# Moving the second layer's down weights out of the second stage of a two-layer split-precision kernel

## The chip, the cores and the metric

The kernel runs on one core of one Trainium2 chip. The time is device microseconds of one execution; three executions of the kernel before are shown, and one more was taken with the hardware profiler. Lower is better.

## The reference

Three parts in a row, all in float32. Tokens are 6080, the model width D is 256, the hidden width FF is 2048.

```python
# gated recurrence over the tokens
sig = 1 / (1 + exp(-f_logit));  f = lower_bound + (1 - lower_bound) * sig
h[t] = f[t] * h[t-1] + (1 - f[t]) * x[t];   y = h
# first layer
h = y @ w_in;   g = h * sigmoid(1.702 * h);   y = g @ w_out
# second layer, its own weights
h = y @ w_in;   g = h if h >= 1, 0 if h <= -1, else (h + 1)**2 / 4;   out = g @ w_out
```

## The kernel before

**Work and tiling.** Each float32 matrix is held as a high part and a remainder, and one float32 product is three matmuls: high by high, high by low, low by high. Tokens are cut in chunks of `WIDTH` columns. `STAGES` lists 12 stages, each one layer on one chunk; they are numbered from 0, so the third stage is stage 2. Stages 0 and 1 are *plain*: the first layer on chunks 0 and 1, 16 steps each (`plain_stage`). Stages 2 to 11 work on pairs of token blocks with a Strassen-like scheme of seven products; each has 8 *groups* (`group(si, g)`), written (stage, group) below, as (2, 5). Stages 2 and 3 are still the first layer; stage 4 is the first of the second layer. A group issues on TensorE (PE) seven up products of three matmuls and eight down half-units of three, 45 matmuls.

**Engines.** PE multiplies. ScalarE (ACT) copies the running sum out of the `chain` bank three times a group (`take`, to `spare`), applies the activation (`act_step`) and rounds it to the high part (`hi_step`, `g_hi`). VectorE (DVE) adds and finishes the activation (`evac`, `g_step`) and makes one remainder of four. GpSimd (POOL) makes the other remainders (`lo_step`, `g_lo`). Every engine runs its instructions in the written order and stops at a semaphore that is not there yet.

**Order beside the groups.** What is not part of a group is hung into it by `fill` functions at fixed places: `fill0`, `fill1`, `fill2` on ACT, places 0 to 3 on DVE and POOL. That work is: the recurrence of the next chunk (`sigmoid_step`, `f_step`, `drive_step`, `last_scan`), the next stage's inputs (`t_sum`, `x_hi`, `x_lo`), and the weights:
- *Block jobs of the second layer* (`more_hi` on ACT, `more_lo` on DVE, then `keep_more` on SP stores them) and *sum jobs* (`weight_sums` on POOL, four small subtractions; `sums_hi` on ACT; `sums_lo` on POOL; `keep_sums` on SP). `SUMS_AT` says at which (stage, step or group) a job stands: jobs 0 to 7 are the first layer's, 8 to 15 the second's. Their raw block is loaded by `load_raw_sums` into one of two buffers in `zout`, and the buffer comes free with `sums_lo` of the job two before.
- *Down weights* (`down_hi` on ACT, `down_lo` on DVE): 8 blocks of each layer, loaded by `load_raw_down` into a quarter of `zraw`. The first layer's are split in stage 0, the second layer's in stage 1, at the steps `DOWN_AT`. They are first used in stage 4.

**Loads.** SyncE (SP) issues all large transfers in one list. In turn g of stage si it comes to `load_weights` for the group two ahead. It waits there for the slot to be free (for a plain stage, two steps' up products of the turn's group; else the group's last chain product) and issues three transfers, the last to `w_a`. PE waits for all three. Around the entry to stage 2 SP has in turn (1, 6): `load_raw_down(1, 7)`, which waits for `down_lo` of block 5, `load_gate(3)` (1 MB), then `load_weights` of (2, 0).

```python
def z_target_free(eng, si, order):
    ...
    if si < 2:
        eng.wait_ge(s_down_dve, down_made(si, NG - 1)[1])
```

The results of stages 0 and 1 go to `zraw` (`z_evac`) and are stored to DRAM (`keep_z`), so that a raw block and a result never share a quarter.

Of the kernel before, what the change touches and what calls it, by code (L numbers as in the profile page):

```python
# [167 lines left out]
def down_buffer(l, g):  # L168

    return g % 2 if l else g % 4  # L170


def down_before(l, g):

    if l == 0:
        return (0, g - 4) if g >= 4 else None
    return (1, g - 2) if g >= 2 else (0, NG - 4 + g)


def down_loads(l, g):  # L180

    return g // 4 + 1 if l == 0 else 2 + g // 2 + 1
# [5 lines left out]
for _g in range(4):  # L188
    SUMS_AT[1, 3 * _g + 1] = _g
    SUMS_AT[2, _g] = 4 + _g  # L190
    SUMS_AT[4, _g] = NG + 4 + _g
for _g in range(2):
    SUMS_AT[2, 4 + _g] = NG + _g
    SUMS_AT[3, _g] = NG + 2 + _g
# [7 lines left out]
DOWN_AT = (0, 2, 4, 6, 8, 13, 14, 15)  # L202
# [14 lines left out]
def build(nc, x, f_logit, lower_bound, w_in0, w_out0, w_in1, w_out1, out):  # L217
    with ExitStack() as ctx:
# [45 lines left out]

        raw_down = [zraw[:, r * 512:(r + 1) * 512] for r in (2, 3, 0, 1)]
# [84 lines left out]
        def z_target_free(eng, si, order):  # L350
# [3 lines left out]
            if si < 2:  # L354
                eng.wait_ge(s_down_dve, down_made(si, NG - 1)[1])
            elif si == 2:
                eng.wait_ge(s_z_kept, 32)
            elif STAGES[si][0] == 0:
# [41 lines left out]
        def _(sp):  # L400
# [33 lines left out]
            def load_raw_down(l, g):  # L434
                before = down_before(l, g)
                if before is not None:
                    by_pool, count = down_made(*before)
                    sp.wait_ge(s_down_pool if by_pool else s_down_dve, count)
# [116 lines left out]
            for G in range(GROUPS):  # L555
# [14 lines left out]
                if si == 1:  # L570
                    if g < 5:
                        load_raw_down(1, g + 2)
                    if g == 5:
                        keep_z(0)
                    if g == 6:
                        load_raw_down(1, 7)
                        load_gate(3)
# [12 lines left out]
                if not is_plain(si):  # L590
                    if SUMS_AT.get((si, g), 0) >= NG:
                        keep_more(SUMS_AT[si, g])
                    kept(si, g)
# [4 lines left out]
                if (si, g) == (0, 7):  # L598
                    load_third(1)
                    load_raw_sums(1)  # L600
                if is_plain(si):
                    kept(si, 2 * g)
                    kept(si, 2 * g + 1)
                if g == 1 and si > 0 and STAGES[si - 1][0] == 1:
# [200 lines left out]
        def _(act):  # L805
# [191 lines left out]
            def fill1(si, g):  # L997
                if si == 2:
# [13 lines left out]
            def fill2(si, g):  # L1012
                if (si, g) in SUMS_AT:
                    sums_hi(SUMS_AT[si, g])
                following = (si, g + 1) if g + 1 < NG else (si + 1, 0)
                if SUMS_AT.get(following, 0) >= NG:
# [575 lines left out]
```

## Time and profile before

| what | value |
|---|---|
| three executions, us | 1026.61, 1028.38, 1030.02 |
| median, us | 1028.38 |
| profiled execution, us | 1029.47 |
| its span, first to last instruction, us | 1027.7 |
| busy PE, DVE, ACT, POOL | 98%, 69%, 70%, 58% of the span |
| mean granted TensorE clock | 0.995 of full |
| chain that ended last | PE 88%, POOL 3%, DMA 3%, issue 2%, ACT 2%, DVE 1% |
| moved by DMA | 133.78 MB |

The profiled execution is 1.77 us longer than its span, and 1.09 us above the median. PE is busy nearly all the time, so what can be lost or won lies in its idle stretches and in stretches at a lower granted clock. Matmul records are drawn 0.39 us long and start every 0.23 us, since they are pipelined: time lost at a stop is the distance between two starts less 0.23.

### The profile page before, as it was taken

What the parts mean: (1) busy time and instruction counts of PE and PEld (TensorE: products, weight loads), DVE (VectorE), ACT (ScalarE), POOL (GpSimd) and SP (SyncE); (2) the same over time, 40 slices, a digit from 0 to 9 for tenths busy, and PEclk for the clock granted to TensorE, in tenths of its full rate; (3) what the DMA queues carried; (4) which work ended last, traced back from release to release, by engine and by line L of the source; (5) the groups of instructions that cost most, each with busy time, mean ns of one, the idle gap of its engine ahead of it and who ended that gap; (6) DMA issues with size and microseconds to landing.
All of it is one profiled execution on the core that took longest, in us unless ns stands there. A gap on an engine that the chain in (4) does not pass through costs nothing.

```text
span 1027.7 us, 14282 instructions
## 1 busy us (share of the span) xinstructions
PE 1010.1 (98%) x4377; PEld 819.5 (80%) x4377; DVE 707.4 (69%) x985; ACT 719.4 (70%) x1334; POOL 596.5 (58%) x476
## 2 busy tenths in 40 slices
PE   8998999999999999999999999999999999999998
PEld 6986878788777888888888888888888888888887
DVE  7773876566797676678667668765456767667766
ACT  7664867666777677677676767766667777776665
POOL 4576777677687347646536655634664673655331
PEclk9998999999999999999999999999999999999999
DMA  9776543722444432232334232223223233423330
GB/s 311 250 243 243 189 173 135 246 97 88 153 174 138 165 124 97 74 105 72 122 140 149 72 104 76 96 84 125 97 74 106 72 108 111 148 73 105 116 108 39
DMA packets 55453, 133.78 MB, mean 130 GB/s; under 512 B 6224, under 2 KB 19152, under 8 KB 54352
## 3 DMA queue, kind: packets, MB, share of 16 engines
q1 hardware_dynamic: 55232, 132.87, 37.0%
q8 instruction: 35, 0.57, 0.2%
q14 instruction: 42, 0.34, 0.1%
q10 hardware_dynamic: 144, 0.00, 0.0%
HBM read 108.86 MB, written 23.99 MB: 129 GB/s over the span
## 4 chain that ended last, share of the span: by engine, by line
PE 88%; POOL 3%; DMA 3%; issue 2%; ACT 2%; DVE 1%; SPq 0%; ACTq 0%; DVEq 0%; POOLq 0%
PE chain L617 24%; PE acc L676 16%; PE acc L672 16%; PE acc L673 16%; PE pair L617 11%; PE single L617 6%; DMA blocks_kept<-zout 1%; POOL g_lo L1470 1%; DMA zout<-w_in_dram 1%; DMA w_a<-blocks_kept 1%; POOL xin1lo L1438 1%; ACT g_hi L956 0%; POOL raw_more L1418 0%; POOL xin0lo L1438 0%; DVE zout L1182 0%
## 5 line engine op out<-in xcount | busy, mean ns | idle before, releaser
L1470 POOL TENSOR_TENSOR g_lo<-g_act,g_hi 128x512 fp32r<-128x512 f32 (+2 forms) x277 | 367.9, 1330 | 400.9 <-ACT g_hi L956 392.4
L916 ACT ACTIVATE spare<-chain 128x512 f32<-128x512 f32 (+1 forms) x264 | 156.8, 594 | 203.5 <-PE chain L617 196.7
L1227 DVE TENSOR_TENSOR spare<-pair,spare 128x512 f32<-128x512 f32 (+1 forms) x176 | 120.9, 687 | 185.6 <-PE pair L617 185.3
L956 ACT ACTIVATE g_hi<-g_act 128x512 fp32r<-128x512 f32 (+2 forms) x277 | 172.9, 624 | 4.2 <-DVE g_act L1251 3.3
L617 PE MATMUL chain<-xin0hi,w_main 128*128 128x512 f32 (+3 forms) x424 | 163.8, 390 | 8.2 <-DMA w_a<-blocks_kept 4.0
L672 PE MATMUL acc<-g_hi,w_down0hi 128*128 128x512 f32 (+1 forms) x384 | 151.0, 393 | 0.9 <-DVE zraw L1215 0.6
L676 PE MATMUL acc<-g_lo,w_down0hi 128*128 128x512 f32 (+1 forms) x384 | 151.2, 394 | 0.1
L673 PE MATMUL acc<-g_hi,w_down0lo 128*128 128x512 f32 (+1 forms) x384 | 150.8, 393 | 0.0
L676 PE MATMUL acc<-g_lo,w_down1hi 128*128 128x512 f32 (+1 forms) x384 | 150.4, 392 | 0.3 <-POOL g_lo L1470 0.3
L672 PE MATMUL acc<-g_hi,w_down1hi 128*128 128x512 f32 (+1 forms) x384 | 150.0, 391 | 0.3 <-DVE zraw L1215 0.3
L673 PE MATMUL acc<-g_hi,w_down1lo 128*128 128x512 f32 (+1 forms) x384 | 150.0, 391 | 0.0
L617 PE MATMUL chain<-xin1hi,w_main 128*128 128x512 f32 x352 | 137.8, 395 | 0.5 <-ACT spare L916 0.5
L1227 DVE TENSOR_TENSOR single<-single,spare 128x512 f32<-128x512 f32 (+1 forms) x88 | 61.1, 695 | 69.8 <-PE single L617 69.6
L617 PEld LDWEIGHTS chain<-xin0hi,w_main 128*128 128x128 f32 x424 | 80.0, 189 | 27.2 <-ACT spare L916 5.7
L949 ACT ACTIVATE g_act<-g_act,one_half 128x512 f32<-128x512 f32 (+1 forms) x96 | 68.6, 715 | 46.3 <-DVE g_act L1238 46.3
L1238 DVE TENSOR_SCALAR g_act<-spare 128x512 f32<-128x512 f32 (+1 forms) x96 | 87.1, 907 | 3.3
L672 PEld LDWEIGHTS acc<-g_hi,w_down0hi 128*128 128x128 f32 x384 | 72.8, 190 | 18.5 <-DVE zraw L1215 1.0
L676 PEld LDWEIGHTS acc<-g_lo,w_down0hi 128*128 128x128 f32 x384 | 72.6, 189 | 17.1 <-POOL g_lo L1470 1.1
L673 PEld LDWEIGHTS acc<-g_hi,w_down0lo 128*128 128x128 f32 x384 | 72.7, 189 | 16.6
L672 PEld LDWEIGHTS acc<-g_hi,w_down1hi 128*128 128x128 f32 x384 | 72.1, 188 | 17.2 <-DVE zraw L1215 0.8
L676 PEld LDWEIGHTS acc<-g_lo,w_down1hi 128*128 128x128 f32 x384 | 72.1, 188 | 16.9 <-POOL g_lo L1470 1.1
L673 PEld LDWEIGHTS acc<-g_hi,w_down1lo 128*128 128x128 f32 x384 | 72.1, 188 | 16.4
(125 smaller groups left out, 1955.4 us busy)
## 6 DMA issues: line engine op xcount, KB each, us to landing
w_main<-sums_kept SPq DMA_DIRECT2D x88, 512.0 KB, 3.6
w_main<-blocks_kept SPq DMA_DIRECT2D x88, 256.0 KB, 3.1
w_a<-blocks_kept SPq DMA_DIRECT2D x88, 128.0 KB, 3.9
sums_kept<-raw_more SPq DMA_DIRECT2D x12, 512.0 KB, 2.9
zout<-w_in_dram SPq DMA_DIRECT2D x20, 256.0 KB, 3.5
out_dram<-zout SPq DMA_DIRECT2D x10, 512.0 KB, 5.6
zraw<-w_out_dram SPq DMA_DIRECT2D x16, 256.0 KB, 5.0
blocks_kept<-w_main SPq DMA_DIRECT2D x8, 512.0 KB, 4.9
```

The lines of the kernel that those rows point to most:

```text
L617: mm = pe.matmul(to, w[a], moving[b], start=start and i == 0, stop=stop and i == 2, skip_group_check=joined)
L672: pe.matmul(to, w[0], g_hi[i][:, 0:n], start=start, stop=False)
L673: pe.matmul(to, w[1], g_hi[i][:, 0:n], start=False, stop=False)
L676: pe.matmul(to, w[0], g_lo[i][:, 0:n], start=False, stop=stop).then_inc(s_unit, 1)
L916: act.activation(snap[k][:, 0:n], chain[g % 2][:, 0:n], ACT.Copy).then_inc(s_snap, 1)
L949: act.activation(t, t, ACT.Square, bias=one_half[:], scale=0.5).then_inc(s_t, 1)
L956: act.activation(g_hi[h % 4][:, 0:n], activated(h), ACT.Copy).then_inc(s_ghi, 1)
L1227: dve.tensor_tensor(to[:, 0:n], bank[:, 0:n], snap[(0, 2, 1)[k]][:, 0:n], ALU.add).then_inc(s_evac, 1)
L1238: dve.tensor_scalar(g_act[i][:, 0:n], hidden_of(h), -1.0, 1.0, ALU.max, ALU.min).then_inc(s_clip, 1)
L1438: pool.tensor_tensor(lo, tile, hi.bitcast(F32), ALU.subtract).then_inc(s_xlo, 1)
L1470: pool.tensor_tensor(g_lo[h % 4][:, 0:n], g_act[h % 4][:, 0:n], g_hi[h % 4][:, 0:n].bitcast(F32), ALU.subtract).then_inc(s_glo_pool, 1)
```

## The change

It touches only the order and the buffers:
- Of the second layer's down weights, blocks 0 and 1 stay in stage 1 (steps 2 and 4). Blocks 2 to 7 are loaded by SP behind the weights in turns (2, 2), (2, 3) and (2, 5), and split one at a time at (2, 4), (2, 5), (2, 6), twice at (2, 7), and (3, 0). Raw blocks now use all four quarters of `zraw`, and the result of stage 2 waits for the last block.
- The gate load of chunk 3 moves from turn (1, 6), ahead of the weights of (2, 0), to turn (1, 5), behind the weights of (1, 7).
- Second-layer jobs 8 and 9 move from (2, 4) and (2, 5) to (2, 5) and (2, 6). Within its group `more_hi` moves from the end of the group before (`fill2`) to the middle of its own (`fill1`), `more_lo` from place 0 to place 2, `weight_sums` of jobs 8 to 15 from place 1 to place 2. For all jobs in groups `sums_hi` moves from `fill2` of the job's group to `fill0` of the next. On SP, `keep_more` comes behind `keep_sums`.
- Inputs of stage 3 (T1, T3 and B22 in stage 2) and of stage 5 (in stage 4) are made up to one group later.

```diff
 def down_buffer(l, g):
-    return g % 2 if l else g % 4
+    return (g + 2 * l) % 4
 ...
 for _g in range(4):
     SUMS_AT[1, 3 * _g + 1] = _g
     SUMS_AT[2, _g] = 4 + _g
+for _g in range(2):
+    SUMS_AT[2, 5 + _g] = NG + _g
+    SUMS_AT[3, _g] = NG + 2 + _g
+for _g in range(4):
     SUMS_AT[4, _g] = NG + 4 + _g
-for _g in range(2):
-    SUMS_AT[2, 4 + _g] = NG + _g
-    SUMS_AT[3, _g] = NG + 2 + _g
 ...
-DOWN_AT = (0, 2, 4, 6, 8, 13, 14, 15)
+DOWN_AT = (2, 4)
+DOWN_HI_AT = ((2, 4, 0), (2, 5, 0), (2, 6, 0), (2, 7, 0), (2, 7, 2), (3, 0, 0))
+DOWN_LO_AT = ((2, 4, 1), (2, 5, 1), (2, 6, 1), (2, 7, 1), (2, 7, 3), (3, 0, 1))
 ...
-        raw_down = [zraw[:, r * 512:(r + 1) * 512] for r in (2, 3, 0, 1)]
+        raw_down = [zraw[:, r * 512:(r + 1) * 512] for r in range(4)]
 ...
             if si < 2:
-                eng.wait_ge(s_down_dve, down_made(si, NG - 1)[1])
+                eng.wait_ge(s_down_dve, down_made(si, (NG - 1, 1)[si])[1])
             elif si == 2:
                 eng.wait_ge(s_z_kept, 32)
+                eng.wait_ge(s_down_dve, down_made(1, NG - 1)[1])
 ...
             def load_raw_down(l, g):
-                before = down_before(l, g)
-                if before is not None:
-                    by_pool, count = down_made(*before)
+                if l == 1 and 2 <= g < 6:
+                    sp.wait_ge(s_z_kept, 32)
+                elif l == 1 or g >= 4:
+                    by_pool, count = down_made(*((0, g - 4) if l == 0 else (0, g + 6) if g < 2 else (1, g - 4)))
                     sp.wait_ge(s_down_pool if by_pool else s_down_dve, count)
 ...
-                if si == 1:
-                    if g < 5:
-                        load_raw_down(1, g + 2)
-                    if g == 5:
-                        keep_z(0)
-                    if g == 6:
-                        load_raw_down(1, 7)
-                        load_gate(3)
+                if (si, g) == (1, 5):
+                    keep_z(0)
 ...
                 if not is_plain(si):
+                    kept(si, g)
                     if SUMS_AT.get((si, g), 0) >= NG:
                         keep_more(SUMS_AT[si, g])
-                    kept(si, g)
 ...
+                if (si, g) == (1, 5):
+                    load_gate(3)
 ...
+                if (si, g) in ((2, 2), (2, 3), (2, 5)):
+                    load_raw_down(1, 2 * (g - 1 - g // 4))
+                    load_raw_down(1, 2 * (g - 1 - g // 4) + 1)
 ...
             def fill1(si, g):
+                if SUMS_AT.get((si, g), 0) >= NG:
+                    more_hi(SUMS_AT[si, g])
 ...
             def fill2(si, g):
-                if (si, g) in SUMS_AT:
-                    sums_hi(SUMS_AT[si, g])
-                following = (si, g + 1) if g + 1 < NG else (si + 1, 0)
-                if SUMS_AT.get(following, 0) >= NG:
-                    more_hi(SUMS_AT[following])
 ...
             def fill0(si, g):
+                if (si, g - 1) in SUMS_AT:
+                    sums_hi(SUMS_AT[si, g - 1])
 ...
+                if (si, g, 0) in DOWN_HI_AT:
+                    down_hi(1, 2 + DOWN_HI_AT.index((si, g, 0)))
 ...
-                if place == 0 and SUMS_AT.get((si, g), 0) >= NG:
+                if place == 2 and SUMS_AT.get((si, g), 0) >= NG:
                     more_lo(SUMS_AT[si, g])
+                if (si, g, place) in DOWN_LO_AT:
+                    down_lo(1, 2 + DOWN_LO_AT.index((si, g, place)))
 ...
-                if place == 1 and (si, g) in SUMS_AT:
+                if (si, g) in SUMS_AT and place == (1 if SUMS_AT[si, g] < NG else 2):
                     weight_sums(SUMS_AT[si, g])
```

**The order on SP at the entry to stage 2.** Before (`w_main1` is the load for group (1, 7), the three rows that end in `w_a220` are those for (2, 0); `zraw` is a raw down block):

```order
L467 DMA z_kept<-zraw 256x1x448
L499 DMA w_main1<-blocks_kept 128x1024
L440 DMA zraw<-w_out1_dram 128x512
L408 DMA gate<-f_logit_dram 128x2048
L502 DMA w_main0<-blocks_kept 128x512
L504 DMA w_main0<-sums_kept 128x1024
L508 DMA w_a220<-blocks_kept 128x256
L480 DMA sums_kept<-raw_more 128x1024
```

Now:

```order
L466 DMA z_kept<-zraw 256x1x448
L498 DMA w_main1<-blocks_kept 128x1024
L405 DMA gate<-f_logit_dram 128x2048
L501 DMA w_main0<-blocks_kept 128x512
L503 DMA w_main0<-sums_kept 128x1024
L507 DMA w_a220<-blocks_kept 128x256
L479 DMA sums_kept<-raw_more 128x1024
```

The raw block is gone from here, and the gate load stands behind the weights of (1, 7), in the turn before.

**The order on ACT at the end of (2, 3) and the start of (2, 4).** Before (`raw_more<-zout` is `sums_hi` of job 7, `zout<-zout` is `more_hi` of job 8):

```order
L916 ACTIVATE spare<-chain1 128x512
L942 ACTIVATE g_act0<-single 128x512
L956 ACTIVATE g_hi3<-g_act3 128x512
L894 ACTIVATE raw_more<-zout 128x4x128
L874 ACTIVATE zout<-zout 128x4x128
L824 ACTIVATE gate<-gate,lb_less_one 128x512
```

Now:

```order
L914 ACTIVATE spare<-chain1 128x512
L940 ACTIVATE g_act0<-single 128x512
L954 ACTIVATE g_hi3<-g_act3 128x512
L822 ACTIVATE gate<-gate,lb_less_one 128x512
L940 ACTIVATE g_act1<-spare 128x512
L954 ACTIVATE g_hi0<-g_act0 128x512
L914 ACTIVATE spare<-chain0 128x512
L954 ACTIVATE g_hi1<-g_act1 128x512
L940 ACTIVATE g_act2<-chain1 128x512
L892 ACTIVATE raw_more<-zout 128x4x128
L878 ACTIVATE w_down1hi<-zraw 128x512
```

`sums_hi` stands six instructions later, down block 2 follows it, and `more_hi` of job 8 has left this place for the middle of (2, 5).

**The order on POOL in (2, 5).** Before, with `weight_sums` of job 9 (four rows `zout<-zout`) ahead of the remainder of tile 3, and one input behind it:

```order
L1408 TENSOR_TENSOR zout<-zout 128x128
L1409 TENSOR_TENSOR zout<-zout 128x128
L1411 TENSOR_TENSOR zout<-zout 128x128
L1413 TENSOR_TENSOR zout<-zout 128x128
L1470 TENSOR_TENSOR g_lo3<-g_act3,g_hi3 128x512
L1438 TENSOR_TENSOR xin1lo<-state,xin1hi 128x512
L1470 TENSOR_TENSOR g_lo0<-g_act0,g_hi0 128x512
```

Now, with those of job 8 behind it:

```order
L1476 TENSOR_TENSOR g_lo3<-g_act3,g_hi3 128x512
L1414 TENSOR_TENSOR zout<-zout 128x128
L1415 TENSOR_TENSOR zout<-zout 128x128
L1417 TENSOR_TENSOR zout<-zout 128x128
L1419 TENSOR_TENSOR zout<-zout 128x128
L1444 TENSOR_TENSOR xin1lo<-gate,xin1hi 128x512
L1476 TENSOR_TENSOR g_lo0<-g_act0,g_hi0 128x512
```

The four subtractions now stand between the remainders of tile 3 and of tile 0.

## Rows read from the trace of the kernel before

**Rows 1.** Who waited for whom, PE, whole span: us in total, times, longest us.
```profile
PE chain L617 <- ACT spare L916: 4.3, 4, 2.2
PE chain L617 <- DMA w_a<-blocks_kept: 4.0, 1, 4.0
PE acc L672 <- DVE zraw L1215: 0.9, 2, 0.6
```
**Rows 2.** Windows: us, busy PE, PEld, DVE, ACT, POOL, then PEclk, DMA share, GB/s.
```profile
80.00:84.00 4.00, 4.00 (x19) 3.25 (x18) 3.02 (x5) 4.00 (x9) 4.00 (x4) 1.00 0.16 67
330.00:1020.00 690.00, 690.00 (x2997) 562.31 (x2996) 471.16 (x664) 485.42 (x899) 364.20 (x268) 1.00 0.29 102
```
**Rows 3.** Timeline of PE around the entry to stage 2: start us, us, instruction, idle before.
```profile
88.79 0.40 PE L676 MATMUL acc<-g_lo,w_down0hi 128*128 128x512 f32 x1
93.18 0.80 PE L617 MATMUL chain<-xin0hi,w_main 128*128 128x512 f32 x1 [4.00 <-DMA w_a<-blocks_kept]
...
98.90 0.46 PE L673 MATMUL acc<-g_hi,w_down0lo 128*128 128x512 f32 x1
```
**Rows 4.** Timeline of SP's queue: raw down block, then first and last load for (2, 0).
```profile
84.04 0.34 SPq L440 DMA_DIRECT2D zraw<-w_out_dram  x1
...
84.96 0.36 SPq L502 DMA_DIRECT2D w_main<-blocks_kept  x1
...
85.84 0.60 SPq L508 DMA_DIRECT2D w_a<-blocks_kept  x1
```
**Rows 5.** Timeline of SP's queue: first load issued in turns (2,3), (2,4), (3,0), (3,1), (4,0), (4,4).
```profile
133.24 0.32 SPq L502 DMA_DIRECT2D w_main<-blocks_kept  x1
...
147.96 0.32 SPq L502 DMA_DIRECT2D w_main<-blocks_kept  x1
...
189.72 0.33 SPq L502 DMA_DIRECT2D w_main<-blocks_kept  x1
...
202.13 0.32 SPq L502 DMA_DIRECT2D w_main<-blocks_kept  x1
...
275.19 0.32 SPq L502 DMA_DIRECT2D w_main<-blocks_kept  x1
...
320.61 0.32 SPq L502 DMA_DIRECT2D w_main<-blocks_kept  x1
```
**Rows 6.** Timeline of ACT: `more_hi` of job 8.
```profile
136.97 0.63 ACT L874 ACTIVATE zout<-zout 128x512 fp32r<-128x512 f32 x1 [1.88 <-DMA zout<-w_in_dram]
```
**Rows 7.** Issues and time to landing: KB, us; window 85.8 to 86.4, then 181 to 183.
```profile
w_a<-blocks_kept SPq DMA_DIRECT2D x1, 128.0 KB, 7.3
...
blocks_kept<-zout SPq DMA_DIRECT2D x1, 512.0 KB, 10.0
```
**Rows 8.** Timeline of PE in (2, 6), an undisturbed group.
```profile
159.61 0.39 PE L617 MATMUL chain<-xin0hi,w_main 128*128 128x512 f32 x1
...
163.53 0.39 PE L676 MATMUL acc<-g_lo,w_down0hi 128*128 128x512 f32 x1
```
**Rows 9.** Timeline of POOL: remainder of tile 3, undisturbed; `weight_sums` twice, first and last of four.
```profile
167.74 1.30 POOL L1470 TENSOR_TENSOR g_lo<-g_act,g_hi 128x512 fp32r<-128x512 f32 x1 [1.88 <-ACT g_hi L956]
...
184.12 0.46 POOL L1408 TENSOR_TENSOR zout<-zout 128x128 f32<-128x128 f32 x1
...
185.61 0.46 POOL L1413 TENSOR_TENSOR zout<-zout 128x128 f32<-128x128 f32 x1
...
74.69 1.44 POOL L1408 TENSOR_TENSOR zout<-zout 128x128 f32<-128x128 f32 x1
...
77.50 0.46 POOL L1413 TENSOR_TENSOR zout<-zout 128x128 f32<-128x128 f32 x1
```
**Rows 10.** By source line: duration ns min/median/max, first and last start us.
```profile
L1470 POOL TENSOR_TENSOR g_lo<-g_act,g_hi x277: 1152/1297/1805, 15.9 to 1014.7; 128x512 fp32r<-128x512 f32 x124, 128x480 fp32r<-128x480 f32 x11, 128x448 fp32r<-128x448 f32 x4
...
L1182 DVE TENSOR_TENSOR zout<-zout x8: 680/1780/1797, 139.4 to 302.0; 128x512 fp32r<-128x512 f32 x8
```

More of the change, by code:

```diff
@@ L168, in down_buffer @@
 def down_buffer(l, g):
-    return g % 2 if l else g % 4
[L173 to L177, printed above, removed]
+    return (g + 2 * l) % 4
 def down_loads(l, g):
-    return g // 4 + 1 if l == 0 else 2 + g // 2 + 1
+    return 2 * l + g // 4 + 1
 SUMS_AT = {}
@@ L1012, in fill2 @@
             def fill2(si, g):
-                if (si, g) in SUMS_AT:
-                    sums_hi(SUMS_AT[si, g])
-                following = (si, g + 1) if g + 1 < NG else (si + 1, 0)
-                if SUMS_AT.get(following, 0) >= NG:
-                    more_hi(SUMS_AT[following])
                 if si + 1 == NS:
                     return
+                if (si, g, 2) in DOWN_HI_AT:
+                    down_hi(1, 2 + DOWN_HI_AT.index((si, g, 2)))
                 if si == 2:
@@ L1022, in fill2 @@
                         f_step(3, g)
-                    if g in (2, 5, 6):
-                        x_hi(3, {2: B21, 5: T3, 6: T4}[g])
+                    if g in (2, 4, 5, 6):
+                        x_hi(3, {2: B21, 4: B22, 5: T3, 6: T4}[g])
                 elif STAGES[si + 1][0] == 1:
@@ L1030, in fill2 @@
                 else:
-                    if 1 <= g <= 3:
-                        x_hi(si + 1, (B11, B22, T3)[g - 1])
-                    if g == 4:
-                        x_hi(si + 1, T4)
+                    late = si == 4
+                    if 1 <= g <= 2:
+                        x_hi(si + 1, (B11, B22)[g - 1])
+                    if 3 <= g - late <= 4:
+                        x_hi(si + 1, (T3, T4)[g - late - 3])
             def fill0(si, g):
+                if (si, g - 1) in SUMS_AT:
+                    sums_hi(SUMS_AT[si, g - 1])
                 if si + 1 == NS:
                     return
+                if (si, g, 0) in DOWN_HI_AT:
+                    down_hi(1, 2 + DOWN_HI_AT.index((si, g, 0)))
                 if si == 2:
-                    if g in (2, 5, 6):
-                        x_hi(3, {2: B11, 5: B22, 6: T2}[g])
+                    if g in (2, 6):
+                        x_hi(3, {2: B11, 6: T2}[g])
                 elif STAGES[si + 1][0] == 1:
@@ L1045, in fill0 @@
                 else:
-                    if g in (2, 3, 4):
-                        x_hi(si + 1, (B21, T1, T2)[g - 2])
+                    late = si == 4
+                    if g == 2:
+                        x_hi(si + 1, B21)
+                    if 3 <= g - late <= 4:
+                        x_hi(si + 1, (T1, T2)[g - late - 3])
             def group(si, g):
@@ L1325, in fill @@
                         last_scan(c)
-                    if g == 2 and place in (1, 3):
-                        t_sum(si + 1, place // 2)
-                    if g == 3 and place == 1:
-                        t_sum(si + 1, 2)
+                    sums = ((3, 3), (4, 1), (4, 3)) if late else ((2, 1), (2, 3), (3, 1))
+                    if (g, place) in sums:
+                        t_sum(si + 1, sums.index((g, place)))
             def group(si, g):
@@ L1504, in fill @@
                 if si == 2:
[L1505 removed]
+                    at = {(3, 0): B11, (3, 2): B21, (5, 0): B22, (5, 2): T1, (6, 0): T3, (7, 0): T2, (7, 2): T4}
                     if (g, place) in at:
@@ L1514, in fill @@
                         x_lo(si + 1, T2)
+                elif si == 4:
+                    at = {(2, 0): B11, (3, 0): B21, (4, 0): B22, (4, 2): T1, (5, 0): T3, (5, 2): T2, (6, 0): T4}
+                    if (g, place) in at:
+                        x_lo(5, at[g, place])
                 else:
```

1 line of the change is left out of this document (removed).

## The prediction

> **What bounds the kernel.** The views were read in this order. The waits of PE come first: three lines hold nearly all of its stops, 4.3 us for ACT's copies of the chain bank in four stops, 4.0 us for one weight transfer, and 0.9 us for the copy of a result out of its accumulator [rows 1]. The windows place them: from 330 to 1020 us PE is busy 690.00 of 690.00 us at full clock [rows 2]. So everything that a change of order can win lies before 330 us, in stages 1 to 4, and the rest is a fixed stream of matmuls, which this change leaves as it is. PE's timeline gives the first stop, the turns in which SP issues weights give the others, because SP issues them when PE ends the last chain product of a group, and so they tick like PE does.
>
> **Entry to stage 2.** The last matmul of stage 1 starts at 88.79 and the first of stage 2 at 93.18 [rows 3]. That is 4.39 us, less the usual 0.23 us between starts: 4.16 us lost. Behind it the granted clock is at the lower of its two levels (1.2 GHz against 2.4), having been full until the stop: 13 matmuls fill 93.18 to 98.90, 5.72 us, where 13 x 0.232 = 3.02 would do. Lost: 2.70 us. Together 6.86 us.
>
> The cause is SP's list. The weights of (2, 0) stand behind a raw down block, which is issued only at 84.04, when DVE has split block 5, and behind the 1 MB gate load; the first weight transfer is issued at 84.96 and the last, `w_a`, at 85.84 [rows 4], and that takes 7.3 us to land [rows 7]. The change takes both away from there. What is late next is the slot: it is free when the up products of step 13 are through, which is 30 matmuls ahead of stage 1's end (six down, then two steps of twelve), so at 88.79 + 0.23 - 30 x 0.232 = 82.06. The issues take 0.88 us as before, so `w_a` leaves at about 83.1 with some 0.2 us of signal. The gate load goes out in the turn before, into a stretch in which the 16 DMA engines are busy only 0.16 of the time [rows 2]. PE wants the weights at 89.02. If `w_a` again took 7.3 us it would land at 90.4, a stop of 1.4 us; but 1.3 MB ahead of it are gone, and I take no stop. Gain 6.86, at worst 5.5.
>
> **The other stops.** A group that nothing disturbs takes (275.19 - 202.13) / 7 = 10.44 us, and four of them 41.76 = 189.72 - 147.96 [rows 5]. The disturbed ones are then: (2, 3) to (2, 4), 14.72 - 10.44 = 4.28; (3, 0) to (3, 1), 12.41 - 10.44 = 1.97; (4, 0) to (4, 4), 45.42 - 41.76 = 3.66 [rows 5]. Sum 9.91 us.
>
> The first is `more_hi` of job 8: ACT stood 1.88 us for its raw block [rows 6], after standing for POOL's `weight_sums`, and PE's copies are behind it on ACT. In the change `more_hi(8)` comes in the middle of (2, 5), about 1.3 groups or 13 us later, while its load is issued in the same turn as before. The 1.88 us are covered seven times. `sums_hi` now waits in the next group, when POOL is long through. The second is `more_hi(11)`, which needs the store of job 10; that landed after 10.0 us, queued behind two 1 MB loads [rows 7]. The store is issued some 3 us later than before, and `more_hi(11)` some 10 us later, so it is covered too. The result copies of (3, 1) and (4, 1) stood behind `more_lo`, 1.78 us on DVE [rows 10], which moves to place 2. The third, in stage 4, is the same pair of waits for jobs 12 to 15 and gets the same two thirds of a group; the inputs of stage 5 also leave (4, 2). I count all 9.91 us as gained.
>
> **What is added.** Six `down_hi`, ACT 0.63 us each (the size of the copy in [rows 6]), and six `down_lo` on DVE, 0.68 us at best, like the subtraction of the same size in [rows 10]. They are removed from stage 1 and stand in (2, 4) to (3, 0). Their cover there is ACT's and DVE's idle time, some 3 us of each 10.44 by their busy shares of 70% and 69% of the span; with that gone a block would cost up to 0.63 + 0.68 us. Their loads come two groups, 21 us, ahead, against 10.0 us for the slowest transfer seen [rows 7]. The new wait of SP for the stored results holds up only the weights of the next turn, which have 7 us. Moving 133.78 MB stays as it is.
>
> The tight place is POOL in (2, 5). The remainder of tile 3 starts 167.74 - 159.61 = 8.13 us after the group's first matmul [rows 8, 9] and ends at 9.43. Now `weight_sums` follows, 1.95 us from the first start to the last end, or 3.27 where DVE is in the way [rows 9], then an input and the remainder of tile 0, each 1.30 (the median) to 1.81 us [rows 10]. End: 13.98 to 16.32. PE wants that remainder 163.53 - 159.61 = 3.92 us into the next group [rows 8], at 14.36. So PE loses between nothing and 1.96 us, once. I take 0.4, near the low end, since DVE is half idle there. Groups without the input end at 12.68 to 14.51: nothing.
>
> **Sum.** 6.86 + 9.91 = 16.77, less 0.4 = 16.4 us. From the profiled execution, 1029.47 - 16.4 = 1013.1. That execution stands 1.09 us above the median; if that is more stopping, it goes with the stops, if not, the result is 1012.0. I say 1013.0.
>
> **A rule that speaks against it.** `more_lo` is one and the same subtraction of 128 x 512 each time, and takes 0.68 us at best and 1.78 in the median [rows 10]; the difference, 1.10, is about one POOL instruction. So DVE and POOL do hold each other up, and the change puts six more such DVE instructions beside a full POOL. The Trainium skill, SBUF — State Buffer, section "Who interferes with whom", says that a VectorE instruction with two SBUF inputs and a GpSimd instruction that reads SBUF exclude each other for the whole instruction, and that whichever issued first wins. By that rule `down_lo` costs a whole instruction of the other engine each time; the trace agrees in size for `more_lo`.
>
> **Rivals.**
> 1. *POOL falls behind* (0.20). For: the place above, and rows of 1.81 us. Against: PE waited for a remainder hardly at all so far. Price: 1.96 us at (2, 6), and I bound the same order of work in stage 4, where ACT has more to do in each group, by as much once more: 1012.7 + 3.9 = 1016.6. This is also where the mutual exclusion leads if every POOL instruction of the gap meets it.
> 2. *A stop stays* (0.10). One of the waits is moved, not removed, or the weights of (2, 0) land late and the clock falls again: 1.4 + 2.7, or 4.28 as at (2, 4): 1013.1 + 4.2 = 1017.3.
> 3. *The change does not do what it says* (0.03). The weights of (2, 0) land no earlier because the gate load is still in flight at 82. Then 6.86 stays lost: 1019.6.
> 4. *Slower* (0.05). ACT now meets six raw down blocks in the middle of first-layer groups. If each arrived after ACT, each would cost what the one late raw block cost, 4.28 us, six times 25.7, against 16.8 won: 1029.5 + 8.9 = 1038. It decides from four late blocks on (17.1). Against: 21 us of lead.
> 5. *No change* (0.02): new stops eat the old.
>
> The forecast itself, 1011.5 to 1015.5, has 0.60.
>
> **How the numbers follow.** The range takes the forecast and rivals 1 to 3: from 1010.3 (the 1012.0 above less 1.7, half the spread of the three runs) to 1019.6. A measurement of this kernel can tell about 0.3%, 3.1 us, from no change. Faster by more is the forecast and rivals 1 to 3: 0.93. Same 0.02, slower 0.05.
>
> **What would show it.** Right: PE's wait for `w_a` gone and the clock 1.00 through 85 to 105 us; `w_a` issued near 83; stage 2's turns 10.44 us apart; ACT's waits for raw blocks and for `weight_sums` gone; PE busy from 330 on as before. Wrong: a wait of PE for POOL's `g_lo` in (2, 6) (rival 1), a clock below 1.00 anywhere after 90 us (rival 2), ACT waiting for `zraw` at (2, 4) to (3, 0) (rival 4).

## The result and the profile after

The changed kernel takes 1013.16 us (median of four runs, 1012.73 to 1013.28), the kernel before 1028.2 beside it (four runs, 1026.61 to 1030.02). The ratio is 0.9852, with a 95% interval of 0.9835 to 0.9869: 15.0 us, 1.5%, faster. The profiled execution took 1013.22 us and its span 1011.4, against 1029.47 and 1027.7.

The profile page of the changed kernel, its head:

```profile
span 1011.4 us, 14282 instructions
...
PE 1003.7 (99%) x4377; PEld 817.4 (81%) x4377; DVE 707.4 (70%) x985; ACT 717.9 (71%) x1334; POOL 597.3 (59%) x476
...
DMA packets 55453, 133.78 MB, mean 132 GB/s; under 512 B 6224, under 2 KB 19152, under 8 KB 54352
```

The same matmuls and the same bytes as before, in 16.3 us less of span. The waits of PE in the changed kernel, whole span (us in total, times, longest us), all of them:

```profile
PE pair L785 <- ACT gate L813: 3.4, 1, 3.4
PE single L615 <- POOL w_main L1405: 0.3, 1, 0.3
PE acc L670 <- POOL w_down0lo L1430: 0.3, 1, 0.3
```

None of the three lines of [rows 1] is left. What is left lies in the start, before 16 us. The timeline of PE at the entry to stage 2, changed kernel (start us, us, instruction), answers to [rows 3]:

```profile
88.82 0.39 PE L674 MATMUL acc<-g_lo,w_down0hi 128*128 128x512 f32 x1
89.05 0.39 PE L615 MATMUL chain<-xin0hi,w_main 128*128 128x512 f32 x1
```

0.23 us between the last matmul of stage 1 and the first of stage 2, where there were 4.39. The windows of the changed kernel (us, busy PE, PEld, DVE, ACT, POOL, then PEclk, DMA share, GB/s) show the clock behind that place, the new load on the DMA engines ahead of it, and the late stages:

```profile
89.20:104.00 14.80, 14.80 (x65) 11.64 (x64) 8.15 (x13) 10.60 (x21) 9.40 (x11) 1.00 0.58 206
80.00:84.00 4.00, 4.00 (x19) 3.21 (x18) 3.04 (x6) 3.49 (x7) 4.00 (x4) 1.00 0.95 355
330.00:1004.00 674.00, 674.00 (x2927) 548.98 (x2926) 460.00 (x649) 474.80 (x879) 356.44 (x263) 1.00 0.29 102
```

The clock stays at full (2.4 GHz) in both windows behind the entry. The stretch in which the DMA engines were busy 0.16 of the time [rows 2] is now at 0.95: the gate load has gone there. SP's queue and the landing of `w_a`, changed kernel, answer to [rows 4, 7]:

```profile
77.43 0.83 SPq L405 DMA_DIRECT2D gate<-f_logit_dram  x1
82.32 0.32 SPq L501 DMA_DIRECT2D w_main<-blocks_kept  x1
...
83.16 0.43 SPq L507 DMA_DIRECT2D w_a<-blocks_kept  x1
```

```profile
w_a<-blocks_kept SPq DMA_DIRECT2D x1, 128.0 KB, 4.9
```

It lands at about 88.1 and PE wants it at 89.05. SP's turns around the old stops of stages 2 and 3 now tick evenly, as the first load issued in (2, 2), (2, 3), (2, 4), (2, 5) and then (3, 0), (3, 1), (3, 2) shows:

```profile
115.89 0.32 SPq L501 DMA_DIRECT2D w_main<-blocks_kept  x1
126.35 0.33 SPq L501 DMA_DIRECT2D w_main<-blocks_kept  x1
136.77 0.33 SPq L501 DMA_DIRECT2D w_main<-blocks_kept  x1
147.23 0.32 SPq L501 DMA_DIRECT2D w_main<-blocks_kept  x1
...
178.81 0.33 SPq L501 DMA_DIRECT2D w_main<-blocks_kept  x1
189.23 0.32 SPq L501 DMA_DIRECT2D w_main<-blocks_kept  x1
199.69 0.32 SPq L501 DMA_DIRECT2D w_main<-blocks_kept  x1
```

10.4 us each; (2, 3) to (2, 4) took 14.72 and (3, 0) to (3, 1) 12.41 before [rows 5]. The two turns left out start at 158.85 and 168.35: (2, 6) is 1.2 us late, SP having waited there for POOL's `sums_lo`, and (2, 7) is back on the beat. PE did not stop for it.

**Where the time came from.** Both traces hold the same 4377 matmuls in the same order, so the start of the n-th can be compared. The distance between the traces grows by 0.32 us late in stage 1, by 4.17 at the entry to stage 2 and by 2.77 in the 13 slow matmuls behind it, by 4.06 in the rest of stage 2 (nearly all at (2, 4)), by 1.90 at (3, 0) to (3, 1), and by 0.52 + 2.96 at the start and in the middle of stage 4. Sum 16.7; the changed execution was 0.36 us later at the start, which leaves 16.3. This is the gain of the profiled execution of the kernel before, a long one; by the medians it is 15.0.

### The profile page after: what moved, and what is told of

The parts are those of the page before. It is cut to its first block, busy times and chain, and to the rows that moved or that the text cites. A ratio compares the mean times of both kernels' runs of the same rounds, so it can differ in the third digit from the quotient of the medians.

```text
span 1011.4 us, 14282 instructions
## 1 busy us (share of the span) xinstructions
PE 1003.7 (99%) x4377; PEld 817.4 (81%) x4377; DVE 707.4 (70%) x985; ACT 717.9 (71%) x1334; POOL 597.3 (59%) x476
## 4 chain that ended last, share of the span: by engine, by line
PE 98%; DMA 0%; POOL 0%; SPq 0%; DVE 0%; issue 0%; ACT 0%; DVEq 0%; POOLq 0%
PE chain L615 26%; PE acc L674 17%; PE acc L671 17%; PE acc L670 17%; PE pair L615 13%; PE single L615 7%; DMA state<-x_dram 0%; POOL w_down0lo L1430 0%; SPq L535 0%; SPq L429 0%; DVE acc L1158 0%; DVE state L1139 0%; DVE zout L1220 0%; ACT w_down0hi L878 0%; ACT xin0hi L827 0%
```

## The experiments

The kernel before ran beside each group: 1027.65 us beside the first four kernels, 1028.74 beside the next four, 1028.13 beside the last three. Theories: (A) the stop at the entry and those at the second-layer jobs are independent, and the change removes each by its own part; (B) one part does it all, since one stop may cause the next; (C) POOL is at its limit after the change.

### The gate load alone

The kernel before, with one edit:

```diff
-                        load_gate(3)
 ...
+                if (si, g) == (1, 5):
+                    load_gate(3)
```

> The kernel before with one edit: the gate load of chunk 3 goes out in turn (1, 5), behind the weights of (1, 7); the raw down block stays ahead of the weights of (2, 0). If both entries of SP's list mattered at the entry to stage 2 (my reading), the weights still leave only after 84.0 us, their last part at about 85.4, and land 3.9 to 6 us later, so PE stops for 0.3 to 2.4 us instead of 4.2 and the clock may or may not fall: 1029.5 - 6.9 + (0.3 to 5) = 1023 to 1027.5 for the profiled execution. Rival, the 1 MB gate load alone was the cause: the stop is gone, 1022.6. Rival, the gate load never mattered: 1029.5, PE's wait for w_a still 4 us. The stops after 100 us (9.9 us together) stay in all three.

Measured: 1024.88 us (ten runs, 1022.56 to 1027.2), ratio 0.9974 (0.9962 to 0.9987). PE's timeline at the entry in this kernel:

```profile
89.10 0.40 PE L677 MATMUL acc<-g_lo,w_down0hi 128*128 128x512 f32 x1
90.60 0.50 PE L618 MATMUL chain<-xin0hi,w_main 128*128 128x512 f32 x1 [1.09 <-DMA w_a<-blocks_kept]
```

The stop is in the expected range; the profiled execution, 1022.56, is a little below the expected 1023 to 1027.5. With the raw down block still ahead of the weights, `w_a` landed in 4.9 us instead of 7.3, and 1.27 us of the 4.16 us stop stayed (1.50 between starts, less 0.23). Behind the shorter stop the matmuls of this execution kept full speed. It is the fastest of the ten, though: three have a mean granted clock of 1.000 and seven 0.998, so in most of them the clock still fell somewhere, and there is no trace that says where. In this trace the gate load ahead of the weights made about 3 us of the stop, and the late issue the rest; by the medians the edit gains 2.8 us.

### The down weights alone, and the whole entry

Two kernels from the one before, both with the new places and buffers of the down blocks; they differ in where the gate load is written. The first:

```diff
-DOWN_AT = (0, 2, 4, 6, 8, 13, 14, 15)
+DOWN_AT = (2, 4)
+DOWN_HI_AT = ((2, 4, 0), (2, 5, 0), (2, 6, 0), (2, 7, 0), (2, 7, 2), (3, 0, 0))
+DOWN_LO_AT = ((2, 4, 1), (2, 5, 1), (2, 6, 1), (2, 7, 1), (2, 7, 3), (3, 0, 1))
 ...
+                if (si, g) == (1, 6):
+                    load_gate(3)
```

The second has these two lines at the end of the turn before instead:

```diff
+                if (si, g) == (1, 5):
+                    load_gate(3)
```

> The kernel before with the down weights moved to stages 2 and 3 as in the change, but the gate load left ahead of the weights of (2, 0) and all jobs and inputs at their old places. SP reaches the gate load when the slot rule lets it, so the weights can leave at 82.3 at once after it, the last part at about 83.7, with 1 MB ahead of them: landing 4 to 7 us later, 87.7 to 90.7, a stop of 0 to 1.7 us without a fall of the clock. 1022.6 to 1024.5 profiled. Rival (the late raw block was harmless, the 1 MB is what counts): a stop near 4 us stays, 1029. If DVE, given six more blocks with the old job places, becomes late in (2, 4) to (3, 0), new stops of some us appear there; my reading says none over 1 us.

> The change with all jobs and inputs put back to their old places: only the down weights and the gate load are moved. My reading: the entry is clean, clock 1.00 through 85 to 105 us, and the stops after 100 us stay: 1029.5 - 6.9 = 1022.6 profiled, 1021.5 to 1022.6 median. PE stops by the profile: 2.2 near 130 us for ACT's copy with a fall of the clock behind it, about 1.1 near (3, 1), about 2.2 in stage 4. Rival (everything later was a consequence of the first stop): the later stops go too, 1013.

Measured: 1022.47 us (five runs, 1021.93 to 1023.38), ratio 0.9953 (0.9938 to 0.9967), and 1021.16 (four runs, 1020.85 to 1021.56), ratio 0.9937 (0.9921 to 0.9953). The expectation for the first was wrong in its mechanism: with the raw block gone nothing stands between the end of turn (1, 5) and the start of (1, 6), and the two kernels issue the same instructions in the same order on every engine. **The gate load is then no edit of its own**; taking the raw block away lets it go out at 77.28. Both kernels came out a little faster than expected (1021.93 and 1020.85 profiled, where at least 1022.6 was said). That two builds of one program differ by 1.3 us is told below.

In both the entry is clean: the first matmul of stage 2 starts at 88.89 and 88.86, at full clock. The later stops stay. PE's waits in the second kernel, after the start:

```profile
PE chain L615 <- ACT spare L914: 3.8, 5, 1.7
...
PE acc L670 <- DVE zraw L1217: 0.9, 2, 0.6
```

They are of the kinds of [rows 1] but for the transfer. One thing was not foreseen. At (2, 4) PE stops twice, 0.96 and 2.05 us between starts and 12 matmuls apart, where the kernel before had one stop of 2.56; together they lose 2.55 us against 2.33, but the clock does not fall behind them. With smaller stops at (3, 1) and in stage 4 that is why this part alone took 8.6 us off the span (1027.7 to 1019.1), and not 6.9.

The two stops also tell what made them. ACT's wait for the raw block of job 8 and its wait before the second stop, in the second kernel, and DVE ahead of that:

```profile
128.31 0.63 ACT L872 ACTIVATE zout<-zout 128x512 fp32r<-128x512 f32 x1 [0.26 <-DMA zout<-w_in_dram]
...
135.18 0.60 ACT L914 ACTIVATE spare<-chain 128x512 f32<-128x512 f32 x1 [2.58 <-DVE spare L1229]
```

```profile
130.72 1.79 DVE L1184 TENSOR_TENSOR zout<-zout 128x512 fp32r<-128x512 f32 x1
132.43 1.78 DVE L1136 SCALAR_TENSOR_TENSOR state<-gate,state 128x512 f32<-128x512 f32 x1
```

The raw block landed in 3.3 us, against 5.0 in the profiled execution of the kernel before, and ACT waited 0.26 us for it in place of 1.88 [rows 6]. It is the same in the kernel with the gate load alone, in the first kernel here and in the one with late inputs below: 3.2 to 3.3 us to landing, a wait of at most 0.26, and still 2.2 to 2.55 us lost at (2, 4). So the loss at (2, 4) does not need the long wait for the raw block. Whether that wait belongs to the kernel before or to its one traced execution is not shown. What is there in all five traces with job 8 at this place is ACT's wait of 2.4 us for `weight_sums`, and `more_lo` with `drive_step` on DVE, 3.5 us in a row, ahead of the sum that ACT's next copy needs.

### The jobs and inputs alone

The changed kernel with the down weights and the gate load as before:

```diff
-DOWN_AT = (2, 4)
+DOWN_AT = (0, 2, 4, 6, 8, 13, 14, 15)
+DOWN_HI_AT = ()
+DOWN_LO_AT = ()
```

> The change with the down weights and the gate load put back: only jobs and inputs are moved. My reading: the entry stop of 4.2 us and the slow clock behind it stay (6.9 us), all later ones go: 1029.5 - 9.9 = 1019.6 profiled, 1018.5 to 1019.6 median; PE waits for w_a 4.0 us and for nothing after 100 us. Rival (the gains overlap, the later stops need the cleaner DMA queue or DVE of the moved down weights): one of the stops near 130, 180 or 290 us stays, 1022 or more.

Measured: 1020.4 us (four runs, 1019.5 to 1021.01), ratio 0.9929 (0.9912 to 0.9945); span 1019.2. The first of PE's waits in this kernel, and the window behind it:

```profile
PE chain L620 <- DMA w_a<-blocks_kept: 4.2, 1, 4.2
```

```profile
94.30:99.00 4.70, 4.70 (x11) 3.73 (x12) 0.00 (x0) 1.12 (x2) 1.84 (x3) 0.50 1.05 424
```

The stop at the entry and the slow matmuls behind it are back, and from 100 us on there is no stop. The time is above the expected 1018.5 to 1019.6: this execution was about 1 us later than that of the kernel before already at 20 us, ahead of anything that was edited. The two parts took 8.6 and 8.5 us off the span, 17.1 together, against 16.3 for the change. By the same-index count the entry's part also saves 1.6 us behind the entry, 1.0 of it at (2, 4), where stage 2 loses 3.0 us in place of 4.06 and the clock does not fall; the jobs' part saves the same again, and the change saves it once. The late start of this execution hides about 1 us of that. Whether the 1.0 us is the edit's or that of one execution is open, since the kernel before has one trace only. Theory A holds but for this piece, B falls.

### One more instruction on POOL in (2, 5)

The changed kernel with a subtraction of 128 x 432 whose result nothing reads:

```diff
+                    if (si, g, place) == (2, 5, 2):
+                        pool.wait_ge(s_xhi, input_n(3, T1))
+                        pool.tensor_tensor(extra[:], column(sums_of(3), 0, 432),
+                                           xin[1][0][:, T1, 0:432].bitcast(F32), ALU.subtract)
```

> The change with one more subtraction of 128 x 432 on POOL at place 2 of (2, 5), into a buffer that nothing reads. It measures whether POOL is at its limit there, which the forecast took as a loss of 0 to 1.96 us and set at 0.4. Such an instruction takes about 1.1 us. My reading (at the limit): PE's matmul on the remainder of tile 0 in (2, 6) starts about 1.1 us later, the whole kernel is 1.0 to 1.3 us longer, the profile shows a wait of PE for POOL's g_lo near 152 us. Rival (POOL has slack there, the small gap of 0.2 us at this place in the changed kernel comes from elsewhere): no such wait, the same span within 0.3 us.

Measured: 1014.97 us (one run), span 1013.2, 1.8 above the change. POOL's timeline and PE's wait in this kernel:

```profile
149.74 0.46 POOL L1420 TENSOR_TENSOR zout<-zout 128x128 f32<-128x128 f32 x1
150.16 1.12 POOL L1513 TENSOR_TENSOR extra<-gate,xin1hi 128x432 f32<-128x432 f32 x1
151.23 1.31 POOL L1445 TENSOR_TENSOR xin1lo<-gate,xin1hi 128x512 fp32r<-128x512 f32 x1
152.50 2.97 POOL L1477 TENSOR_TENSOR g_lo<-g_act,g_hi 128x512 fp32r<-128x512 f32 x2
```

```profile
154.27 0.51 PE L675 MATMUL acc<-g_lo,w_down0hi 128*128 128x512 f32 x1 [1.55 <-POOL g_lo L1477]
```

1.95 us between starts at this place, where the changed kernel has 0.44. An instruction of 1.12 us cost 1.5 us, more than the expected 1.0 to 1.3: POOL has no slack there. The other 0.4 us come from DVE. The remainder of tile 0 now starts at 152.50, when `down_lo` runs on DVE (152.18 to 153.09), and takes 1.72 us; in the changed kernel it starts first, at 151.20 against 151.98, and takes 1.29. (C) is right for this one place.

### `sums_hi` of jobs 4 to 7 back in its old place

```diff
             def fill2(si, g):
+                if SUMS_AT.get((si, g), NG) < NG:
+                    sums_hi(SUMS_AT[si, g])
 ...
-                if (si, g - 1) in SUMS_AT:
+                if SUMS_AT.get((si, g - 1), 0) >= NG:
```

> The change with sums_hi of the first layer's jobs 4 to 7 back at the end of their own group, where ACT stands for POOL's weight_sums (5.2 us in three waits before). My reading: these waits come back, 1 to 2.4 us each, but the stop of PE at (2, 4) was made by the wait for the raw block that followed on top; alone they are covered: no stop above 0.3 us, 1013 to 1013.5. Rival (the waits for POOL were what used up ACT's lead): a stop of PE of 1 to 2.5 us comes back near 126 us, 1014 to 1018.

Measured: 1014.66 us (four runs, 1014.45 to 1015.07), ratio 0.9859 (0.9842 to 0.9875), 1.5 above the change. ACT's wait from 88 to 320 us in this kernel is back, but PE's only new stop stands elsewhere:

```profile
ACT raw_more L892 <- POOL zout L1421: 4.1, 2, 2.4
```

```profile
153.76 0.51 PE L674 MATMUL acc<-g_lo,w_down0hi 128*128 128x512 f32 x1 [0.85 <-POOL g_lo L1478]
```

Neither my reading nor its rival had this. The wait on ACT costs PE 0.6 us in small gaps at 128 to 134 us and delays the work behind it, and that arrives at (2, 6), where POOL has no slack.

### `more_hi` back at the end of the group before

```diff
             def fill1(si, g):
-                if SUMS_AT.get((si, g), 0) >= NG:
-                    more_hi(SUMS_AT[si, g])
 ...
             def fill2(si, g):
+                following = (si, g + 1) if g + 1 < NG else (si + 1, 0)
+                if SUMS_AT.get(following, 0) >= NG:
+                    more_hi(SUMS_AT[following])
```

> The change with more_hi back at the end of the group before (fill2), while more_lo stays at place 2 of its own group. My reading: more_hi then needs the store of the job before, which now leaves only some 8.7 us into the group and takes 5 us and more, so ACT stands about 5 us at jobs 9, 11, 13, 14 and 15; PE stops at each for 3 us or more, and the clock falls after the longer ones: 10 to 27 us lost, 1023 to 1040. So the places of more_hi and more_lo are one edit. Rival (the place of more_hi alone decides nothing): 1013 to 1014.

Measured: 1024.93 us (one run), span 1023.1: 11.7 us above the change, worse than any part left out. ACT's waits, whole span, and PE's two long stops in this kernel:

```profile
ACT zout L872 <- DMA blocks_kept<-zout: 15.2, 5, 4.1
```

```profile
282.69 0.50 PE L615 MATMUL chain<-xin0hi,w_main 128*128 128x512 f32 x1 [2.55 <-ACT spare L914]
...
296.18 0.80 PE L615 MATMUL chain<-xin0hi,w_main 128*128 128x512 f32 x1 [2.80 <-ACT spare L914]
```

`more_hi` overwrites a buffer that the store of the job before still reads. That store follows `more_lo`, and `more_lo` now stands at place 2, later in its group. So a `more_hi` at its old place meets a later store, and ACT stands up to 4.1 us. **The places of `more_hi` and `more_lo` are one edit**: the one moved without the other costs most of the gain.

### Inputs of stage 5 at their old places

The changed kernel with `late = 0` on ACT, the earlier table of sums on DVE and without POOL's late table; of the diff, ACT's and POOL's part:

```diff
-                    late = si == 4
+                    late = 0
 ...
-                elif si == 4:
-                    at = {(2, 0): B11, (3, 0): B21, (4, 0): B22, (4, 2): T1, (5, 0): T3, (5, 2): T2, (6, 0): T4}
-                    if (g, place) in at:
-                        x_lo(5, at[g, place])
```

> The change with the inputs of stage 5 (t_sum on DVE, x_hi on ACT, x_lo on POOL in stage 4) back at their old, up to one group earlier, places. In the kernel before, stage 4 lost about 3.5 us. My reading: most of that was ACT standing for raw blocks and stores, so with the jobs moved only a little returns, 0 to 1 us, from DVE and POOL full in (4, 2): 1013 to 1014. Rival (crowding by the inputs was the cause in stage 4): 2.5 to 3.5 us return, 1015.7 to 1016.7, with PE waiting for ACT's copies near 290 us.

Measured: 1016.75 us (four runs, 1016.47 to 1016.93), ratio 0.9877 (0.9857 to 0.9898). That is 3.6 us above the change, where I had expected 0 to 1; the rival had the size right, but PE waits for POOL and not for ACT's copies. PE's timeline at two places of stage 4, and POOL's ahead of the first, in this kernel:

```profile
291.06 0.50 PE L674 MATMUL acc<-g_lo,w_down1hi 128*128 128x512 f32 x1 [1.44 <-POOL g_lo L1476]
...
302.52 0.50 PE L674 MATMUL acc<-g_lo,w_down1hi 128*128 128x512 f32 x1 [0.74 <-POOL g_lo L1476]
```

```profile
285.53 0.64 POOL L1414 TENSOR_TENSOR zout<-zout 128x128 f32<-128x128 f32 x1
...
288.29 1.30 POOL L1444 TENSOR_TENSOR xin1lo<-state,xin1hi 128x512 fp32r<-128x512 f32 x1
289.56 3.15 POOL L1476 TENSOR_TENSOR g_lo<-g_act,g_hi 128x512 fp32r<-128x512 f32 x2
```

`weight_sums` at place 2 and an input's remainder stand in one gap of POOL, in (4, 2) and in (4, 3), and behind each the remainder of tile 0 comes late. Stage 4 lost 3.1 us; the other 0.5 are a late `w_a` at the entry (PE waited 0.72 us for it in this execution).

### Inputs late, jobs as before

The second kernel of the entry with the late inputs of stage 5 added (the reverse of the diff above), to see whether the inputs alone do it:

> The kernel of e3 (down weights and gate load moved, all jobs at their old places) with the inputs of stage 5 moved as in the change. It asks whether stage 4's loss of about 3.4 us goes with either edit alone: with the jobs moved and the inputs not, it stayed at 3.1. My reading now: both are needed, since ACT still stands for raw blocks at the old job places: 1.5 to 3 us of the 3.4 stay, median 1020 to 1021. Rival (the inputs alone crowd stage 4, the jobs don't matter there): PE has no stop after 265 us, 1017.8 to 1018.3.

Measured: 1022.49 us (1021.13, 1020.57, 1024.98, 1023.86), ratio 0.9942 (0.9919 to 0.9965). The median is above the expected 1020 to 1021, and the runs lie too far apart to tell it from the 1021.16 without the input move. The trace can: of the 3.3 us (0.54 + 2.78) that stage 4 lost in that kernel against the change, 2.9 stay, with stops like this one:

```profile
294.44 0.50 PE L615 MATMUL chain<-xin0hi,w_main 128*128 128x512 f32 x1 [1.40 <-ACT spare L914]
```

So in stage 4 neither edit is enough by itself: with only the inputs moved 2.9 us stay lost, with only the jobs moved 3.1.

### T1 one place earlier, and the change again

One input's remainder leaves the full gap of POOL in (2, 5); beside it the changed kernel once more:

```diff
-                    at = {(3, 0): B11, (3, 2): B21, (5, 0): B22, (5, 2): T1, (6, 0): T3, (7, 0): T2, (7, 2): T4}
+                    at = {(3, 0): B11, (3, 2): B21, (5, 0): B22, (5, 1): T1, (6, 0): T3, (7, 0): T2, (7, 2): T4}
```

> The change with the x_lo of input T1 in (2, 5) moved from place 2 to place 1 on POOL, where POOL idles 2.0 us before the remainder of tile 3. Its source is ready by then (x_hi of T1 ends about 1.5 us before). My reading: the gap of PE at the remainder of tile 0 in (2, 6), 0.2 us over the usual distance, is gone, and 1.3 us of room are there: median 1012.9, 0 to 0.5 us below the change's. Rival: x_lo at place 1 comes before x_hi is done, POOL's remainder of tile 3 is late instead: 1013.5 to 1015.

> The change itself again, beside e10 on the same chip, to see how far executions of it differ. Two of the kernels that enter stage 2 in the same way showed PE stopping 0.7 and 1.1 us for the last weight transfer, two others did not. My reading: the transfer's landing has less than 1 us of room, so the median lies between 1012.7 and 1014 and executions differ by up to 1.5 us. Rival: the spread is that of the first result, 0.6 us.

Measured: 1013.16 us (four runs, 1012.55 to 1013.98) and 1013.29 (four runs, 1012.92 to 1014.05), ratios 0.9852 (0.9835 to 0.9869) and 0.9852 (0.9837 to 0.9867). The gap at (2, 6) is gone, and what PE loses in small gaps after 89 us falls from 0.77 to 0.46 us, but the median is not below the change's: 0.3 us cannot be told from run to run. The repeat of the change shows a wait that the first execution had not:

```profile
PE chain L615 <- DMA w_a<-blocks_kept: 0.5, 1, 0.5
```

So the changed kernel itself can stop at the entry. Of the two stops that the expectation names, the one of 1.1 us was the kernel with the gate load alone, which does not enter stage 2 in the same way; the one of 0.7 was the kernel with old inputs.

## Why the prediction was right

Forecast 1013.0, measured 1013.16; for the profiled execution 1013.1, measured 1013.22.

**The entry, 6.86.** The stop and the slow clock both went, the next matmul followed after 0.23 us. The same-index count gives 4.17 for the stop and 2.77 for the slow matmuls: 6.9. The issue of `w_a` came at 83.16, forecast about 83.1. The landing took 4.9 us, which puts it 1 us ahead of PE. "I take no stop" was in part luck: in the ten traces with this order on SP the same transfer took 4.9 to 6.7 us, 6.0 in the median, with 5.9 us of room here. Where it took 6.5 and 6.7 us (the repeat, and the kernel with old inputs) PE waited 0.5 and 0.7 us for it, and the clock did not fall. My counting of the gate load as a part of its own was wrong, since it moves by itself once the raw block is gone; where the raw block stays, moving it was worth about 3 us of the stop in the one trace.

**The other stops, 9.91.** 4.06 + 1.90 + 3.48 = 9.4 by the same-index count, in which the 0.3 us on POOL are already taken off: forecast 9.91 less 0.4. No ACT wait for a raw block, a store or `weight_sums` is left from 88 to 320 us; the longest total is the copies' own wait for their products, changed kernel:

```profile
ACT spare L914 <- PE chain L615: 41.4, 44, 2.4
ACT g_act L947 <- DVE g_act L1243: 6.0, 6, 1.2
```

Three steps were told too simply. The 4.28 us at (2, 4) were put on ACT, which stood for `weight_sums` and then 1.88 us for the raw block. In the four other traces with job 8 at this place the wait for the raw block is at most 0.26 us and PE still loses 2.2 to 2.55 us, behind `weight_sums` and behind `more_lo` and `drive_step` on DVE, which the sum left out. The number held because the change moves all of them apart. Only the wait for `weight_sums` was put back by itself; it cost 1.5 us. For stage 4 I named the pair of waits and gave the input move a half sentence; each alone leaves about 3 us of the 3.3 lost. And "covered seven times" spoke of the load that `more_hi` waits for; its second wait, for the store of the job before, is what the place of `more_lo` sets, and with the one moved alone it cost 11.7 us.

**POOL, 0.4.** The gap at (2, 6), changed kernel:

```profile
152.11 0.40 PE L671 MATMUL acc<-g_hi,w_down0lo 128*128 128x512 f32 x1
152.55 0.50 PE L674 MATMUL acc<-g_lo,w_down0hi 128*128 128x512 f32 x1
```

0.2 us there and 0.1 behind it. The sum of durations from [rows 9, 10] put POOL's end between 13.98 and 16.32 us against a need at 14.36; an added 1.12 us that cost 1.5 shows that it stood at the edge. (The 14.51 us of the groups without the input is 0.15 over that need, and not nothing, but no such stop is seen.) The mechanism of rival 1 is real: it appeared in three kernels (added instruction, old `sums_hi`, old inputs), and the change escapes it in stage 4 by its later inputs.

**The rule that spoke against it.** The six moved `down_lo` take 1.00 us in the median beside a fuller POOL, within 0.72 to 1.61, and PE shows no stop for them; the added instruction above shows what one can cost where POOL has no slack. The feared side fell out the other way for `more_lo`. For job 8, in the kernel before it started 0.04 us after an instruction of POOL, and took 1.78; in the change it falls in POOL's idle time. DVE and POOL of the kernel before, then of the changed one:

```profile
139.37 1.78 DVE L1182 TENSOR_TENSOR zout<-zout 128x512 fp32r<-128x512 f32 x1
...
139.33 2.96 POOL L1470 TENSOR_TENSOR g_lo<-g_act,g_hi 128x512 fp32r<-128x512 f32 x2 [2.40 <-ACT g_hi L956]
```

```profile
145.19 0.67 DVE L1187 TENSOR_TENSOR zout<-zout 128x512 fp32r<-128x512 f32 x1
...
146.14 1.49 POOL L1476 TENSOR_TENSOR g_lo<-g_act,g_hi 128x512 fp32r<-128x512 f32 x1 [2.02 <-ACT g_hi L954]
```

Seven of eight `more_lo` took 1.77 to 1.80 us before; five of eight take 0.68 now and three 1.18. The Trainium skill, SBUF — State Buffer, section "Who interferes with whom", says that a VectorE instruction with two SBUF inputs contends with a GpSimd instruction that reads SBUF, that the port pair they share is an exclusive lock, and that issue order decides who is blocked. The trace agrees for these rows. Of POOL's two instructions before, the first, ahead of DVE, ran from 139.33 to 140.60, 1.27 us; DVE's ended 0.55 us after it; and the second, which started at 140.56, took 1.73. So moving an instruction by half a group shortened it by 1.1 us.

**Rivals 2 to 5** did not come in the profiled execution: no stop over 0.5 us after 16 us, the entry's weights in time, no ACT wait for `zraw`, and the 1.09 us by which the profiled execution before stood above its median went with the stops. Of rival 2 the late landing was seen in the two other traces named above, without its price. The kernel before varies by 3.4 us over its four runs and the changed one by 0.6. The granted clock goes some way with that. Of the 28 executions of the kernel before beside the experiments, 14 have a mean clock of 0.998 and a median of 1027.4 us, nine 0.997 and 1028.9, three 0.996 and 1028.1, and two 0.995 and 1031.1; the profiled one has 0.995. So the profiled execution paid more slow matmuls than most. The forecast took this in by its two bases, 1013.1 and 1012.0; the measured 1013.16 fits a surplus that was stops and slow matmuls.

## What to carry to other kernels

When PE is busy at full clock over most of the span, list its few stops, trace each to the one instruction that an in-order engine or queue holds in front of the work PE needs, and price it as the stop plus the slow matmuls behind it. Moves that share a buffer or a gap are one edit: test them together, since the one left behind can cost most of the gain (11.7 us here). Look at the same stop in a second trace before naming its cause: here the longest wait ahead of it was gone in four other kernels, and the stop was not. After a change that works, look for the next tight place (here POOL in (2, 5) and 1 us of room for `w_a`), since the next edit will meet it.

## What was not expected of the hardware

**A stop's length alone does not say whether the clock falls.** Between starts, stops of 2.56 (kernel before, at (2, 4)), 3.20 (old `more_hi`), 4.39 and 4.54 us were followed by 8 to 13 matmuls at 0.43 us each, the 1.2 GHz level; stops of 1.77, 1.95, 2.05 and 2.95 us were not. These are stops of profiled executions. So 2.56 us dropped the clock in one place and 2.95 did not in another. The windows behind the two, first of the kernel before, then of the kernel with `more_hi` in its old place:

```profile
140.00:143.50 3.50, 3.50 (x9) 2.75 (x9) 3.50 (x4) 0.73 (x2) 3.50 (x3) 0.51 0.38 151
```

```profile
282.70:285.00 2.30, 2.30 (x10) 1.91 (x11) 1.31 (x2) 2.30 (x5) 2.09 (x3) 1.00 0.01 4
```

PE starts again at 139.78 and at 282.69, so both windows lie wholly behind their stops. What decides stays open here. For a prediction it means that a stop between 2 and 3 us should be given both prices; the slow matmuls at (2, 4) cost about 8 x 0.2 = 1.6 us.

**One program, two builds, 1.3 us.** The two entry kernels issue the same instructions in the same order, and their runs do not overlap (1020.85 to 1021.56 and 1021.93 to 1023.38). The traces put the difference in ACT's copies (3.8 and 4.8 us of PE's wait for them), above all at (3, 0), where only the slower one stops for 1.53 us, and not in the entry. Why was not found; differences of this size between kernels that still have stops prove nothing by themselves.

**A small transfer's landing moves with what is ahead of it, and from execution to execution.** `w_a`, 128 KB, takes 4.0 us in the median of the changed kernel's 88. At the entry it took 7.3 and 7.4 us in the two traces with 1.3 MB issued just ahead of the weights. With the gate load out 6 us before it took 4.9 to 6.7 us in ten traces, and the two of the unchanged program, 4.9 and 6.5, are nearly as far apart. So a room of 1 us at such a place should be priced as a stop that comes in some executions.
